# Packed attention and two dense layers on one core: a schedule with loops and GpSimd work, rewritten as one straight-line plan

## The reference

```
for b in 8 batches, 8 heads:                      # q, k, v: 576 x 64, p: 32 x 64
    p_packed = softmax(p @ k.T / 8) @ v           # first attention, 32 x 64
    x = softmax(q @ p_packed.T / 8) @ p_packed    # second attention, 576 x 64
x = x as 4608 tokens x 512
h = x @ w_in                                      # 512 -> 2048
y = (max(h, 0) + alpha * min(h, 0)) @ w_out       # 2048 -> 512, "leaky" step
out = (silu(y @ w_gate) * (y @ w_val)) @ w_out2   # 512 -> 1536 -> 512
```

## Time and profile before

| | |
|---|---|
| median of 3 runs | 1769.65 us (1769.49 to 1769.89) |
| profiled execution, its span | 1767.1 us |
| start (to the first L692 of slot 0) | 93.5 us |
| phase 1 (from there to the L692 of slot 255) | 791.8 us |
| phase 2 and end | 881.8 us |
| PE busy | 1681.6 us, 95% |
| DVE, ACT, POOL busy | 932.4, 575.4, 293.8 us |

### The profile page before, as it was taken

One profiled execution on the slowest core, in us unless ns is written; L12 is line 12 of the kernel. 1 busy time (PEld: TensorE's weight loads), 2 busy tenths in 40 slices (PEclk: granted clock), 3 DMA queues, 4 the chain that ended last, 5 costly groups with the idle time before them and its releaser, 6 DMA issues.

```text
span 1767.1 us, 26368 instructions
## 1 busy us (share of the span) xinstructions
PE 1681.6 (95%) x9424; PEld 1489.1 (84%) x9424; DVE 932.4 (53%) x1638; ACT 575.4 (33%) x1337; POOL 293.8 (17%) x265
## 2 busy tenths in 40 slices
PE   5699998999989999999999999999999999999998
PEld 4489997899979998899988888888888888888887
DVE  6788778878788788977642323222222222222322
ACT  6664456544564446634520101010101101010100
POOL 3534333434334334310000000000000000000000
PEclk7599999999999999999999999999999999999999
DMA  5422122122222122212320101010100001010000
GB/s 171 147 66 67 48 84 88 41 74 76 72 78 73 56 55 86 77 37 86 98 85 1 48 1 48 0 47 0 38 9 14 33 0 47 0 47 0 24 1 24
DMA packets 53918, 90.56 MB, mean 51 GB/s; under 512 B 5664, under 2 KB 22064, under 8 KB 53808
## 3 DMA queue, kind: packets, MB, share of 16 engines
q1 hardware_dynamic: 51472, 79.71, 14.4%
q0 software_dynamic: 2336, 9.45, 1.4%
HBM read 70.26 MB, written 18.87 MB: 50 GB/s over the span
## 4 chain that ended last, share of the span: by engine, by line
PE 82%; DVE 10%; issue 4%; ACT 3%; DMA 0%; POOL 0%; DVEq 0%; ACTq 0%; SPq 0%; POOLq 0%
PE acc L688 12%; PE h L563 8%; PE h L565 8%; PE h L564 8%; PE side L563 8%; PE side L565 7%; PE side L564 7%; PE acc L692 6%; PE acc L565 6%; PE acc L563 6%; PE acc L564 6%; DVE floats L1087 3%; DVE operands L984 2%; DVE operands L1093 2%; ACT operands L773 2%
## 5 line engine op out<-in xcount | busy, mean ns | idle before, releaser
L984 DVE TENSOR_TENSOR operands<-floats,operands 128x288 fp32r<-128x288 f32 (+2 forms) x498 | 325.4, 665 | 71.0 <-ACT operands L773 58.2
L688 PE MATMUL acc<-operands 128*128 128x288 f32 x2048 | 321.5, 298 | 36.9 <-DVE operands L1093 30.2
L688 PEld LDWEIGHTS acc<-operands 128*128 128x128 f32 x2048 | 283.9, 188 | 53.8 <-DVE operands L1093 36.8
L563 PE MATMUL h<-operands 128*128 128x288 f32 (+1 forms) x944 | 320.9, 340 | 0.0
L564 PE MATMUL h<-operands 128*128 128x288 f32 (+1 forms) x944 | 319.5, 338 | 0.0
L565 PE MATMUL h<-operands 128*128 128x288 f32 (+1 forms) x944 | 319.4, 338 | 0.0
L563 PE MATMUL side<-operands 128*128 128x512 f32 (+3 forms) x696 | 264.2, 380 | 30.7 <-DVE operands L984 25.7
L520 POOL TENSOR_TENSOR operands<-floats,operands 128x288 fp32r<-128x288 f32 (+2 forms) x194 | 219.0, 1129 | 342.3 <-ACT operands L773 333.8
L564 PE MATMUL side<-operands 128*128 128x512 f32 (+3 forms) x696 | 257.6, 370 | 0.0
L565 PE MATMUL side<-operands 128*128 128x512 f32 (+3 forms) x696 | 257.4, 370 | 0.0
L1087 DVE SCALAR_TENSOR_TENSOR floats<-floats 128x288 f32<-128x288 f32 x256 | 166.6, 651 | 102.1 <-ACT floats L879 100.0
(11 more groups left out here) (53 smaller groups left out, 1689.1 us busy)
## 6 DMA issues: line engine op xcount, KB each, us to landing
floats<-w_in SPq DMA_DIRECT2D x64, 256.0 KB, 2.5
floats<-kT SPq DMA_DIRECT2D x64, 144.0 KB, 2.2
floats<-qT SPq DMA_DIRECT2D x64, 144.0 KB, 2.1
y_scratch<-floats POOLq DMA_DIRECT2D x16, 576.0 KB, 3.5
floats<-y_scratch SPq DMA_DIRECT2D x9, 1024.0 KB, 5.0
out<-floats SPq DMA_DIRECT2D x36, 256.0 KB, 2.3
floats<-vS SPq DMA_DIRECT2D x32, 256.0 KB, 2.9
floats<-w_out SPq DMA_DIRECT2D x16, 256.0 KB, 3.0
```

The lines of the kernel that those rows point to most:

```text
L563: pe.matmul(dst, w[0], x[0], start=start, stop=False, **kw)
L688: pe.matmul(acc[m][:, 0:CH], w2[:, j, x, m * P:(m + 1) * P], g[:, s % 2, 0, :], start=j == 0 and x == 0, stop=False)
L984: return nc.vector.tensor_tensor(dst, x, high.bitcast(F32), ALU.subtract)
```

## The change

Nearly every line is rewritten. The arithmetic that reaches the output is the same up to the form of the leaky step. What is different:

1. **No hardware loops.** One list `PLAN` holds all events of phase 1 for all 256 slots, written out; every engine walks it once. Phase 2 is written out too.
2. **Start.** `START_A` does only the first attention of batch 0, its second attention for the first 288 tokens (`scores2 0 0`), and the first quarter of its mix. Then slot 0 begins. The rest of batch 0, and batch 1, go into slots 0 to 33.
3. **Mixes of batches 0 and 1 apart** (`mixA`, 12 matmuls of 512 columns for each quarter of `w_in`, with the other batch's rows of `both` zeroed), and `w_in` loaded and split for each. Pairs 1 to 3 are mixed two batches at once, as before.
4. **Leaky step.** ACT makes `Relu(-h)` (one instruction instead of two), DVE makes `gF = (1 - alpha) * Relu(-h) + h`, reading h from PSUM (L1028); the high part of `g` is now a copy on ACT (L716) instead of a CAST on DVE; the subtraction stays on DVE.
5. **Order within a slot.** `h` is two slots ahead of `y` instead of one. `PLAN` has for slot s: `g(s+1)` (ACT high part, DVE low part), the events `FRONT`, the events `MID` (splits, exponentials), `h(s+2)`, the first event of `BACK`, `gF(s+2)`, the rest of `BACK`, `y(s)`.
6. **No arithmetic on GpSimd.** DVE makes all low parts and both steps of the second softmax. POOL keeps three kinds of memset and the stores of y.
7. **Splits just in time**: k and q pieces are 576 wide (two halves in one), put into `MID` at most 3 slots ahead of their use; `split_p` stands in the slot before `scores1`.
8. **max1 and exp1** read the scores from PSUM; `scores1` is written by 12 matmuls in one slot instead of two times 6, and `scores2` too.

```
+PLAN = list(START_A)
+for _s in range(SLOTS):
+    if _s + 1 < SLOTS:
+        PLAN.append(("g", _s + 1))
+    PLAN += FRONT[_s] + MID[_s]
+    if _s + 2 < SLOTS:
+        PLAN.append(("h", _s + 2))
+    elif _s + 1 == SLOTS:
+        PLAN.append(("gate", 0, 0))
+    PLAN += BACK[_s][:1]
+    if _s + 2 < SLOTS:
+        PLAN.append(("gF", _s + 2))
+    PLAN += BACK[_s][1:]
+    PLAN.append(("y", _s))
...
+    MID[max(0, min(max(_free, _s - 3), _s - 1))].append(("split", _p))
...
+    _s = [s for s in range(SLOTS) if ("scores1", _b, 0) in FRONT[s]][0]
+    MID[_s - 1].append(("split_p", _b))
...
-            def relus(it, s):
...
-                nc.scalar.activation(pos[:, s % 2, :], hb[s % 2][:, 0:CH], ACT.Relu)
-                nc.scalar.activation(neg[:, s % 2, :], hb[s % 2][:, 0:CH], ACT.Relu, scale=-1.0
-                                     ).then_inc(relu_done, 1)
+            def neg(s):
+                once.wait_ge(h_done, s + 1)
+                once.wait_ge(g_split, s - 1)
+                nc.scalar.activation(gF[:, s % 2, :], hb[s % 2][:, 0:CH], ACT.Relu, scale=-1.0).then_inc(neg_done, 1)
+            def g_hi(s):
+                once.wait_ge(gF_done, s + 1)
+                once.wait_ge(y_done, s - 1)
+                copy(g[:, s % 2, 0, :], gF[:, s % 2, :]).then_inc(g_high, 1)
+            def g_float(s):
+                once.wait_ge(neg_done, s + 1)
+                j = s % NT1
+                nc.vector.scalar_tensor_tensor(out=gF[:, s % 2, :], in0=gF[:, s % 2, :], scalar=alphas[:, j:j + 1],
+                                               in1=hb[s % 2][:, 0:CH], op0=ALU.mult, op1=ALU.add
+                                               ).then_inc(gF_done, 1)
+            def g_lo(s):
+                once.wait_ge(g_high, s + 1)
+                subtract(g[:, s % 2, 1, :], gF[:, s % 2, :], g[:, s % 2, 0, :]).then_inc(g_split, 1)
-            def split(it, p):
...
-                nc.gpsimd.tensor_tensor(piece[k, slot, 1, 0:n], raw[k, slot, 0:n],
-                                        piece[k, slot, 0, 0:n].bitcast(F32), ALU.subtract).then_inc(raw_split, 1)
```

More of the change, by code:

```diff
@@ L47 @@
 ST = (SEQ + P - 1) // P
-BLK = SEQ // PACK
+BLK = CH // PACK
 SCALE = float(D) ** -0.5
 EPS = 1e-9
[L52 to L73, removed]
@@ L103, in _softmax2 @@
[L103 to L120, removed]
@@ new lines, in _second_attention @@
+def _second_attention(b, c, at):
+    FRONT[at].append(("scores2", b, c))
+    BACK[at].append(("turn2", b, c))
+    BACK[at + 1].append(("max2", b, c))
+    MID[at + 2].append(("exp2", b, c))
+    BACK[at + 2].append(("sum2", b, c))
+    BACK[at + 3].append(("norm2", b, c))
+for _n in range(1, 4):
+    for _half in range(2):
+        FRONT[3 * _n - 3 + _half].append(("mixA", 0, _n, _half))
+BACK[8].append(("rezero", 0))
+_second_attention(0, 1, 6)
+BACK[12].append(("attn", 0, 1))
+_first_attention(1, 9)
@@ new lines, with before, mixes_before, mixed_by @@
+PLACE = {e: n for n, e in enumerate(PLAN)}
+MIXES = [e for e in PLAN if e[0] in ("mix", "mixA")]
+MIX_NO = {e: n for n, e in enumerate(MIXES)}
+def before(e, kind):
+    return sum(x[0] == kind for x in PLAN[:PLACE[e]])
+def mixes_before(e):
+    return sum(x[0] in ("mix", "mixA") for x in PLAN[:PLACE[e]])
+def mixed_by(b, n):
+    last = ("mixA", b, n, 1) if b < 2 else ("mix", b // 2, n, KD - 1)
+    return MIX_NO[last] + 1
+PIECES = [e[1] for e in PLAN if e[0] == "split"]
+PIECES += [("x", n) for n in range(len(WEIGHT_SLOT), 3 * NT2)]
@@ L757, in chunk @@
+            for c in range(NC2):
                 for j in range(NT2):
@@ L960, in chunk @@
-            def chunk(c, last=False):
+                    if c == 0:
+                        once.wait_ge(y_stored, 16 * NCH)
+                    once.wait_ge(out_stored[m], 16 * c)
+                    copy(ostage[:, m, :], acc[:, m, :]).then_inc(out_copied[m], 1)
+            for e in PLAN:
+                if e[0] == "split":
+                    split(e[1])
+                elif e[0] == "split_p":
+                    split_p(e[1])
+                elif e[0] == "exp1":
+                    exp1(e)
+                elif e[0] == "turn":
+                    turn(e)
+                elif e[0] == "spread":
+                    spread(e[1])
+                elif e[0] == "packedT":
+                    packedT(e[1])
+                elif e[0] == "exp2":
+                    exp2(e)
+                elif e[0] == "mixA":
+                    mix_a(e)
+                elif e[0] == "mix":
+                    mix(e)
+                elif e[0] == "attn":
+                    attn_c(e)
+                elif e[0] == "h":
+                    neg(e[1])
+                elif e[0] == "g":
+                    g_hi(e[1])
+                elif e[0] == "ycopy":
+                    y_copy(e[1])
+                elif e[0] == "yin":
+                    y_part(0, e[2])
+                elif e[0] == "gate":
+                    silu(0, 0)
```

1430 lines of the change are left out of this document (704 added, 726 removed), and 3 rows, old and new, of the table START_A.

## The result

The changed kernel takes **1799.6 us** (median of 4 runs, 1799.5 to 1800.5), the kernel before 1769.6 us in runs beside it: ratio 1.0178, 95% interval 1.0163 to 1.0192. It is slower by 30 us. I had forecast 1782, slower by 12. Direction and range (1742 to 1806) hold; the size does not.

What follows compares the result with a forecast made beforehand. It took TensorE as the bound, 99% busy in phase 2 and waiting 68 us in phase 1. The sum 1767.1 - 37.5 + 22.1 - 68 + 96 = 1779.7 gave 1782 us as median of runs, range 1742 to 1806.

Steps and rivals of the forecast that it cites:

- The start: Before slot 0: with one batch's chain it shrinks from 93.5 to 56 us, a gain of 37.5 us.
- Side work on TensorE, +22.1: Phase 1: matmuls and a packing moved in from the start, 10.0 us, more mixes, 12.9, one h tile fewer, -0.8.
- Waits that go, 68: Phase 1: all 68 us of TensorE's old waits vanish without GpSimd arithmetic and loops.
- Waits that come, 96: Phase 1: new TensorE waits, 38 us in mix runs, 47 in batches 1 to 7, 11 elsewhere.
- the ring: Each slot: gF on DVE, ACT's copies, DVE's subtractions, next gF must turn once; 4.0 us in mix slots, 1.4 in empty ones.
- The clock falls in the new waits: Rival, phase 1: eight to ten waits of 3.5 us or more halve the clock, +17, 1799 us; chance 0.13.
- Mix slots: Phase 1: 4.0 us each after four slots of a run, against 3.07 of TensorE work; three runs pay 14 + 12 + 12.
- Slot 101: Phase 1: `scores1` waits for p's split, 4 + 3.65 - 2.39 = 5.5 us of TensorE wait.
- the seven batches: Phase 1, batches 1 to 7: TensorE waits 9, 5, 6, 5, 7, 7, 7, given as 47 us.
- the handovers of `acc`: Phase 1: sixteen handovers where y waits for lagging DVE and ACT; with slots 6, 7, 26 to 28 and 209, 11 us.
- The lead covers the ring: Rival, phase 1: TensorE's lead of two h tiles hides the ring; waits 52 instead of 96, 1738 us; chance 0.27.
- Loads bind in slots 0 to 12: Rival, early phase 1: 29 pieces through four raw buffers take 1.4 us each, +9, 1791 us; chance 0.10.

Runs made afterwards that it cites:

- the version without waits: Changed kernel with g's high part on VectorE, p's split three slots ahead and pieces' low parts on GpSimd; its mix runs are free of waits: 1737.2 us.

## Why the prediction was wrong in size

*The start.* 56 us forecast, 52.9 measured, 40.6 us gained instead of 37.5. Right, and mis-sized by 3 us.

*Side work on TensorE, +22.1.* 5483 matmuls in phase 1 against 5352, 131 more. Right: the matmuls priced by shape give 22.4 us, and mix slots without waits last 3.07 us, as the forecast's work per slot had it.

*Waits that go, 68.* Right that they go. The kernel before with the leaky step alone shows that 34.6 us of them leave without any of the rest.

*Waits that come, 96.* **This is the step that failed.** The sum was priced at full clock throughout. The total is 116.6 us: 95.7 of waits, which the ring's sum met, and 20.9 of matmuls at half clock behind them, which it left out. I had them as a rival ("The clock falls in the new waits", +17, 1799 us, chance 0.13) and set it low since one wait of before had left the clock full. It was right in kind: eleven stretches, 1.9 us each, where it had eight to ten. That they are a cost of their own and not hidden in the ring's lag is shown at four places by the added matmuls, 6.6 to 7.7 us; for the other 13 to 14 it is the sum of spacings, not a run. With the rival's term the forecast's sum, 1782 + 17, is the measured time; part of that closeness is luck, since the start was 3 us better than forecast.
The Trainium skill ("TensorE: Matmul & The Clock Gate", Part 1) says that an idle TensorE loses its full clock and has it back after activity; slot 101 agrees, with 0.59 granted behind 3.62 us of wait and 1.00 ahead of it.

*Place by place* the waits hold less well than their sum. Mix slots turn in 4.16 to 4.25 us, not 4.0, and the run of slots 120 to 136 took 67.0 us where the version without waits took 51.6: 15.4 instead of 12. Slot 101 lost 5.4 us as forecast (5.5), but by 3.9 of wait and 1.5 of clock. The 5.5 was also mis-added: 4 + 3.65 - 2.39 is 5.3, and the lag that its own slots 95 to 99 give is 3.4 us, not 4, which makes 4.6. The list of the seven batches adds up to 46, not 47. And the waits for the handovers of `acc` are 17.0 us (9.6 and 7.4 in the table) where 11 was to cover them and more. That the errors cancel is chance.

*The other rivals.* "The lead covers the ring" falls: the lead of two h tiles covered the first four slots of a run (3.07 each) and no more, as the forecast itself said. "Loads bind in slots 0 to 12" stays small: ScalarE waits 2.2 us for loads there, 3.1 in the second run of the same code, whose slots 2 to 6 took 2.5 us longer.

*What the change's parts are worth.* Leaky step: -34.6 us, measured alone. From there to the changed kernel +65: the start gives 40 and takes 22 back as side work, so the new waits with their clock cost some 83 more than the 33 that the kernel with the leaky step alone still had (757.2 us of phase 1 less 723.8). Undone in the changed kernel, g's copy on ScalarE is worth 58, the pieces' subtractions on VectorE 41, the place of the leaky step in the slot 31; these overlap and are not to be added.

## What to carry to other kernels

Sum the ring, not the engine: an instruction that waits for another engine and stands first in an in-order queue puts everything behind it into the chain, and 256 copies of 0.45 us, one a slot, became 58 us although ScalarE was half idle. Price the longer waits of TensorE twice, once as a wait and once as the matmuls behind it at half clock; in this kernel the second part came to a fifth of the first, though of the waits of about 2 us four left the clock full. Take a rewrite apart before judging it: the part with no order in it, one Relu and one SBUF input less, was faster by 34.6 us alone.

## What the runs showed of the hardware that was not expected

GpSimd at work does not slow every VectorE instruction alike. Two SBUF inputs: 457 to 542 ns and 758 to 1155; one of them in PSUM: 500 and 501, 688 and 688. But it also slows a copy with a single SBUF input, the CAST of 288 columns, from 308 to 450 ns, which the forecast did not have, though the kernel before shows it too: 485 ns from 150 to 710 us, 310 from 800 to 880.
The Trainium skill ("GPSIMD Engine Reference", section 1) names both kinds, two SBUF inputs and the two-port performance mode; the trace agrees with the first by those rows, and if the CAST of 308 ns ran in that mode, which no row shows, with the second.

Matmuls whose result nobody reads, placed wholly inside four waits, made those slots 6.6 to 7.7 us shorter (the medians fell by 2.5 and by 9.6 us in two pairs of runs); placed behind a wait of their own, they cost 2.4 to 4.7 us a place.
